# VectorE's first six weight differences put behind GpSimd's twelfth scatter, two of them among the row differences

## What is computed

```python
# attention, per step t: state S, output y
S_re, S_im = (new_re + kv, new_im)
y[:, :, t] = np.einsum('bhd,bhde->bhe', q[:, :, t], S_re)
...
# experts: each token's row goes to the next free slot of its expert
expert_idx = np.argmax(logits, axis=1)
...
h = np.maximum(np.einsum('ecd,edf->ecf', disp, w1), 0.0)
y = np.einsum('ecf,efd->ecd', h, w2)
...
# dense network
h = x @ w_in
g = np.maximum(h, 0.0) + alpha * np.minimum(h, 0.0)
return (g @ w_out).astype(np.float32)
```

## Time and profile before

| | before |
|---|---|
| median of 3 runs | 523.41 us (521.82 to 523.44) |
| the profiled execution, its own time | 521.51 us |
| its span, first to last instruction | 519.5 us |
| PE busy | 453.2 us, 87% |
| DVE busy | 347.5 us, 67% |
| ACT busy | 270.2 us, 52% |
| GpSimd busy | 43.2 us, 8% |

### The profile page before, as it was taken

One profiled execution on the slowest core, in us unless ns is written; L12 is line 12 of the kernel. 1 busy time (PEld: TensorE's weight loads), 2 busy tenths in 40 slices (PEclk: granted clock), 3 DMA queues, 4 the chain that ended last, 5 costly groups with the idle time before them and its releaser, 6 DMA issues.

```text
span 519.5 us, 9890 instructions
## 1 busy us (share of the span) xinstructions
PE 453.2 (87%) x3712; PEld 409.6 (79%) x3712; DVE 347.5 (67%) x551; ACT 270.2 (52%) x425; POOL 43.2 (8%) x50
## 2 busy tenths in 40 slices
PE   0539999999930499999999989999999999999995
PEld 0327788899920499999999988999989999899994
DVE  2589898863260377767777776877747787478750
ACT  5999998573450366666666653343333333343312
POOL 3000000000047800000000000000030000200002
PEclk9969999999965599999999999999999999999999
DMA  8980000100023786576666672332333333220001
GB/s 320 423 351 2 5 3 3 3 3 3 3 71 137 258 276 190 188 220 198 203 196 186 197 220 87 94 119 91 92 121 107 106 96 109 92 70 1 0 1 63
DMA packets 27149, 63.75 MB, mean 123 GB/s; under 512 B 7894, under 2 KB 9430, under 8 KB 27100
## 3 DMA queue, kind: packets, MB, share of 16 engines
q1 hardware_dynamic: 25564, 58.34, 35.0%
q0 software_dynamic: 1536, 4.74, 2.4%
HBM read 58.28 MB, written 4.76 MB: 121 GB/s over the span
## 4 chain that ended last, share of the span: by engine, by line
PE 82%; DVE 5%; POOL 3%; DMA 3%; issue 3%; ACT 2%; SPq 0%; POOLq 0%; DVEq 0%; ACTq 0%
PE banks L1285 17%; PE banks L1283 17%; PE banks L1284 16%; PE banks L1293 8%; PE banks L1067 4%; PE banks L1294 4%; PE banks L1022 3%; POOL rows_by_slot L389 3%; PE banks L1090 2%; PE banks L1053 2%; PE banks L1093 2%; PE banks L1056 2%; PE banks L1103 1%; DMA th<-a_im_rows 1%; PE banks L1277 1%
## 5 line engine op out<-in xcount | busy, mean ns | idle before, releaser
L942 DVE TENSOR_TENSOR w_lo<-raw_early,w_hi 128x768 fp32r<-128x768 f32 x84 | 80.0, 957 | 30.4 <-ACT w_hi L597 29.4
L642 ACT ACTIVATE g_hi<-g_all 128x512 fp32r<-128x512 f32 x48 | 30.4, 634 | 118.7 <-DVE g_all L995 116.3
L597 ACT ACTIVATE w_hi<-raw_early 128x768 fp32r<-128x768 f32 x84 | 70.5, 844 | 31.9 <-PE banks L1294 31.7
L1283 PE MATMUL banks<-w_hi,g_hi 128*128 128x384 f32 x192 | 65.1, 339 | 0.5 <-DVE g_lo L997 0.5
L1285 PE MATMUL banks<-w_hi,g_lo 128*128 128x384 f32 x192 | 65.0, 339 | 0.0
L1284 PE MATMUL banks<-w_lo,g_hi 128*128 128x384 f32 x192 | 64.9, 338 | 0.0
L1293 PE MATMUL banks<-h_hi_lo,w_hi 128*128 128x448 f32 x192 | 63.9, 378 | 0.4 <-DVE h_hi_lo L958 0.4
L997 DVE TENSOR_TENSOR g_lo<-g_all,g_hi 128x512 fp32r<-128x512 f32 x48 | 33.3, 693 | 44.3 <-ACT g_hi L642 44.3
L1283 PE MATMUL banks<-ys_hi,w_hi 128*128 128x512 f32 x144 | 56.1, 389 | 1.4 <-DVE ys_lo L972 1.4
L1285 PE MATMUL banks<-ys_hi,w_lo 128*128 128x512 f32 x144 | 57.1, 397 | 0.0
L1284 PE MATMUL banks<-ys_lo,w_hi 128*128 128x512 f32 x144 | 56.8, 395 | 0.0
(11 more groups left out here) (146 smaller groups left out, 934.0 us busy)
## 6 DMA issues: line engine op xcount, KB each, us to landing
raw_early<-weights SPq DMA_DIRECT2D x84, 384.0 KB, 3.6
raw_late<-weights SPq DMA_DIRECT2D x28, 384.0 KB, 3.0
xq<-q_rows SPq DMA_DIRECT2D x3, 776.0 KB, 16.7
xq<-rows_by_slot SPq DMA_DIRECT2D x12, 194.0 KB, 4.2
kk<-k_rows SPq DMA_DIRECT2D x3, 768.0 KB, 18.1
vv<-v_rows SPq DMA_DIRECT2D x3, 768.0 KB, 19.5
aa<-a_re_rows SPq DMA_DIRECT2D x2, 768.0 KB, 10.6
th<-a_im_rows SPq DMA_DIRECT2D x2, 768.0 KB, 12.0
```

The costliest lines, as they stand in the source:

```text
L597: A(wh[:, slot, :], raw[slot], ACT.Copy).then_inc(w_hi, 1)
L642: A(gh[:, c % GBUF, :], gg[:, c % GBUF, :], ACT.Copy).then_inc(g_hi, 1)
L942: TT(wl[:, slot, :], raw[slot], wh[:, slot, :].bitcast(F32), ALU.subtract).then_inc(w_lo, 1)
L1283: MM(o, lhsT=whi, rhs=mhi, start=first, stop=False)
```

## The change

The change touches three places.

1. A new semaphore `issued`. GpSimd's program increments it behind the twelfth scatter and ahead of the two fills. The increment is an instruction of its own (an event on a semaphore), not attached to a scatter.
2. DVE waits for `issued` ahead of its first weight difference, and makes only four of them there (`FIRST` = 4).
3. The weight difference of chunk 4 stands behind the eighth row difference, that of chunk 5 behind the tenth.

```diff
@@ GpSimd
                 pool.indirect_dma_start(xs_dram, bass.IndirectOffsetOnAxis(ap=slots_i[:, t:t + 1], axis=0),
                                         xq[:, x:x + XW], None).then_inc(scattered, 16)
+            pool.sem_inc(issued, 1)
             pool.memset(yh[:, :, :].bitcast(F32), 0.0)
             pool.memset(yl[:, :, :].bitcast(F32), 0.0).then_inc(cleared, 1)
@@ VectorE
-            for r in range(AHEAD):
+            dve.wait_ge(issued, 1)
+            for r in range(FIRST):
                 split_lo(r, r)
             for r in range(NT):
+                if r >= NT - 2 * (AHEAD - FIRST) and r % 2 == 0:
+                    i = AHEAD - (NT - r) // 2
+                    split_lo(i, i)
                 dve.wait_ge(row_hi, r + 1)
```

More of the change, by code:

```diff
@@ L66, in fused_attention_moe_mlp @@
     AHEAD = RING - 2
+    FIRST = 4
     PARTS = NF + 1
@@ L198, in fused_attention_moe_mlp @@
         many_ready, slotted, bases = sem("many_ready"), sem("slotted"), sem("bases")
-        scattered = sem("scattered")
+        scattered, issued = sem("scattered"), sem("issued")
         row_dma = [sem(f"row_dma{i}") for i in range(NT // LOAD_ROWS)]
```

## The result

The changed kernel takes **518.84 us** (median of 6 runs, 517.9 to 519.22), before took 523.33 on the same chip: a ratio of 0.9923, with a 95% interval of 0.9909 to 0.9936. On another chip a repeat gave 518.75 against 521.85, 0.9937 (0.9918 to 0.9956). The quotient of the two medians is 0.9914 on the first chip and 0.9941 on the second. The changed kernel is faster by 3 to 4.5 us. The forecast was 522.7 and its range began at 519.8.

The account below looks back on a forecast made before the run. It took PE as the bound behind a chain of waits through the scatters. 521.5 - 1.4 (scatters) + 0.7 (rows) = 520.8 us profiled; by the median 523.4 - 0.7 = 522.7 us, range 519.8 to 524.2.

Parts of the forecast that it names:

- The increment comes early: On GpSimd's sequencer: `issued` is incremented while an earlier scatter is at work, so the next scatter starts amid four differences.
- five or eight fit: Cases of how many scatters GpSimd's sequencer hands over ahead: with five or eight, the increment comes during the fourth to seventh.
- only one: Case where GpSimd's sequencer can hand over only one scatter ahead: the increment comes still during the eleventh.
- p: Time in us from a scatter's start to the start of DVE's four differences; taken as 0.4, from 0.1 to 1.27.
- my formula: Time lost at the scatters to four gapless differences, p + 2.16 us: 2.6 expected, 2.3 to 3.4 possible, against 4.01 before.
- the sign of being right: In POOL's timeline: one scatter among the first to eleventh takes 3.3 to 4.4 us, with four differences beside it.
- 0.7 us lost: At the row differences: two moved weight differences make PE wait about 0.6 us, plus 0.1 for the clock; bounds 0.4 and 1.0.
- The clock: TensorE's clock rise stays put while rows come 1.4 us earlier, so two more tiles run slower; 0.1 us booked.
- The first rival: The wait works and no scatter is blocked: scatters end 4.0 us earlier; 518.2, or 520.1 by the median; chance 0.14.
- The slow rival: POOL's two fills hold the four differences until they end: +2.4 us, 523.9, or 525.8 by the median; chance 0.05.
- The sum: Whole profiled execution: 1.4 us gained at the scatters, 0.7 lost at the rows, 521.5 to 520.8 us.

Follow-up runs that it names:

- g1: The kernel before with an event (wait for `consts`) and a 128x1 fill on DVE between `base_i` and the six differences; 520.08 us, before at 523.34.
- g2: The kernel before with an event straight ahead of its six differences, and GpSimd's first scatter also waiting for `bases`; 521.48 us, before at 523.34.

## Why the prediction was wrong, point by point

- **The increment comes early: right.** "If all can be handed over at once, during the first": it came at 151.8, even ahead of the first scatter's start, so the cases in which five or eight fit, or only one, are out. The rule that I cited (the Trainium skill, PSUM — Partial Sum Buffer, Engine vs sequencer instructions) held. The differences began at p = 0.12, not at the 0.4 that I took. By my formula that is 2.28 us lost in place of 2.6, and 0.3 us of the miss.
- **"A loss of p + 2.16": the step that failed.** It was made of "a scatter is held while differences run without a gap", read from one kernel, and is exact for a program without the event: 2.28 in the run without the wait. I priced the wait by its moment alone and never asked what the added event does on DVE. With it each end of a difference lets a scatter in. No scatter of the changed kernel took the 3.3 to 4.4 us that I had named as the sign of being right. The loss was 1.02 us with four differences and 1.49 with six. That is 1.3 us of the miss.
- **"0.7 us lost" at the rows: mis-sized, it is 0.** I had named a PE that does not wait at `output(0)` as the sign of it. PE came to `output(0)` 3.11 us behind its first hidden product, before and after. The timeline of DVE and PE in the changed kernel:

```profile
180.78 0.95 DVE L944 TENSOR_TENSOR w_lo<-raw_early,w_hi 128x768 fp32r<-128x768 f32 x1
181.65 1.01 DVE L955 TENSOR_TENSOR xs_lo<-banks,xs_hi 128x384 fp32r<-128x384 f32 x2
182.58 0.38 DVE L964 SCALAR_TENSOR_TENSOR h_hi_lo<-banks,h_hi_lo 128x224 fp32r<-128x224 f32 x1
...
L992 DVEq SEQ_ASSERT  x1: 35/35/35, 181.3 to 181.3; - x1
...
183.14 0.38 PE L1299 MATMUL banks<-h_hi_lo,w_hi 128*128 128x448 f32 x1
```

  The last row difference did end later, 182.66 - 180.03 = 2.63 us behind PE's first hidden product, before 1.01: 1.62 of the 1.74 that I booked. But the load of the row number and the branch, which I put behind it at 0.5 us, were through at 181.6, while DVE was still at the last weight difference and had two row differences to go. The low part was there at 182.96, 0.2 us ahead of PE. Before, too, the load had begun ahead of the last row difference's start (183.2), so I was wrong to put this work behind its end:

```profile
L986 DVEq TENSOR_LOAD <-base_i x1: 549/549/549, 183.1 to 183.1; - x1
```

- **The clock: the 0.1 us booked for it was not lost.** I let the rise stay where it was. The granted clock rose from 0.50 to 1.00 in the 177 to 178 us slice here, 3 us earlier than before, along with the rows, again behind some 3 us of transposes without a gap (the clock is the third column from the end):

```profile
177.00:178.00 1.00, 1.00 (x8) 0.67 (x7) 0.92 (x2) 0.91 (x3) 0.64 (x1) 0.85 1.02 376
```

  From the last scatter's start to the first hidden product it took 13.1 us, before 13.2.
- **The first rival** (518.2, 520.1 by the median) had the right size for a wrong reason: no difference was behind the scatters. Made to be true, its mechanism gave 518.1 to 518.5, or 0.993 of before, as its 520.1 is of 523.4 (0.994). **The slow rival** fell there as well: 951 ns for a difference beside a fill, against 940, and g1 and g2 have 951 without a fill.
- **The sum.** By the profiles, -3.0 at the scatters and 0 at the rows, where I had -1.4 and +0.7. That is the size of the 3.1 us of the second chip. Of the 4.5 us between the medians of the first, 1.4 remain unexplained; by the ratio of 0.9923 the gain there is 4.0 us (3.3 to 4.8), and before's six runs spread over 1.7 us.
- **What went wrong in weighing.** I gave the forecast its own range from the bounds of p, that is, from one formula, as if the formula were sure. It rested on one held scatter.

## What to carry to other kernels

A semaphore increment of its own behind a queue of transfers says only that they were handed over; to wait for their end on the issuing engine, attach it to a small instruction behind them. A second wait on an instruction is an instruction too, and may change how another engine's work gets in beside it even where it never waits: take it alone, and compare the held instruction's length, before believing the reason written beside it. And a price read from a single contended instruction holds for the program it was read in.

## What the runs showed of the hardware that was not expected

- A GpSimd indirect transfer that starts in a run of two-input DVE instructions (0.94 us each, 0.87 apart) ends 0.83 to 0.84 us (the first of twelve 0.99) behind either the end of the one it met or the end of the whole run; the two programs that were profiled twice had the same pattern both times. With an event on DVE's sequencer between the instruction ahead of the run and the run it is the former, in eight of eight profiles: 1.35 to 1.44 us where nothing else was changed, in place of 3.09 (four) or 4.83 (six). Without one it is the latter, in seven of seven. Why is not shown.
- The same event ahead of the third instruction of the run, or one instruction too early, has no effect: 4.83 us, in one profile each.
- GpSimd's sequencer passed all twelve transfers before the first began (event at 151.8, first scatter at 152.02).
- The first of twelve transfers takes 1.11 us with no weight difference beside it, the others 0.96.
